# The first pair of heads in a fused attention and feed-forward kernel: an earlier projection, low parts read from the PSUM bank, two copies made by transfer, and the next pair's splits spread over four groups

## What is computed

```python
def _attn_ref(q, k, v, proj):                 # q, k, v: (2, 8, 768, 64), proj: (64, 6)
    q_bits = (np.einsum('bhsd,dk->bhsk', q, proj) > 0).astype(np.int64)
    k_bits = (np.einsum('bhsd,dk->bhsk', k, proj) > 0).astype(np.int64)
    powers = 2 ** np.arange(n_bits)
    q_bucket = np.sum(q_bits * powers, axis=-1)
    k_bucket = np.sum(k_bits * powers, axis=-1)
    mask = q_bucket[:, :, :, None] == k_bucket[:, :, None, :]
    scores = scale * np.matmul(q, k.transpose(0, 1, 3, 2))
    scores = np.where(mask, scores, -1000000000.0)
    attn = softmax(scores)                    # written out with max, exp and sum in the original
    return np.matmul(attn, v)

def reference(...):
    x = attention output as (B * S, H * D)    # (1536, 512)
    x = max(x @ w1, x @ w2, x @ w3) @ w_out
    h = x @ w_in
    return (h / (1 + exp(-1.702 * h))) @ w_out2
```

## Time and profile before

| | us |
|---|---|
| median of 3 runs | 678.75 |
| lowest, highest | 678.73, 679.58 |
| the profiled execution, its own time | 679.09 |
| its span, from the first to the last instruction | 677.3 |
| mean granted clock of TensorE | 0.997 |

### The profile page before, as it was taken

How to read it: one execution, slowest core, us unless ns; L and a number is a source line. 1 busy time by engine, 2 the same in 40 slices (tenths; PEclk the granted TensorE clock), 3 DMA queues, 4 the chain that set the end, 5 groups by cost and what they waited for, 6 DMA issues and landing times.

```text
span 677.3 us, 11910 instructions
## 1 busy us (share of the span) xinstructions
PE 664.4 (98%) x3867; PEld 575.4 (85%) x3867; DVE 494.7 (73%) x981; ACT 345.9 (51%) x758; POOL 473.0 (70%) x532
## 2 busy tenths in 40 slices
PE   7799999999999999999999999999999999999998
PEld 5677777777777789999999999998888989888886
DVE  5877778787878799869778952778777665555554
ACT  5777877777867731011102453456454555445433
POOL 4756746688876799977871628798888667777720
PEclk8999999999999999999999999999999999999999
DMA  5736638457253101111001200112222224221102
GB/s 139 168 85 158 147 87 184 120 128 166 64 140 119 32 4 44 48 32 31 24 27 45 94 0 32 63 62 66 89 80 80 63 66 152 63 63 62 40 23 94
DMA packets 58268, 53.97 MB, mean 80 GB/s; under 512 B 28608, under 2 KB 47200, under 8 KB 58208
## 3 DMA queue, kind: packets, MB, share of 16 engines
q1 hardware_dynamic: 56560, 52.82, 29.1%
q10 hardware_dynamic: 1648, 0.39, 0.3%
HBM read 32.51 MB, written 3.15 MB: 53 GB/s over the span
## 4 chain that ended last, share of the span: by engine, by line
PE 89%; POOL 5%; DVE 2%; DMA 1%; issue 1%; ACT 1%; ACTq 0%; DVEq 0%; POOLq 0%
PE psS L1434 10%; PE psO L1456 10%; PE psR L1442 9%; PE psR L1503 7%; PE psR L1504 7%; PE psR L1505 7%; PE psS L1503 6%; PE psS L1505 6%; PE psS L1504 6%; PE psS L1604 4%; PE psS L1603 4%; PE psS L1602 4%; POOL w_lo L690 2%; PE psR L1384 1%; POOL w_raw L681 1%
## 5 line engine op out<-in xcount | busy, mean ns | idle before, releaser
L549 POOL TENSOR_SCALAR probs<-probs,lone,inv 128x768 f32<-128x768 f32 x96 | 93.9, 985 | 62.2 <-DVE inv L1071 62.2
L690 POOL TENSOR_TENSOR w_lo<-w_raw,w_hi 128x256 fp32r<-128x256 f32 x96 | 79.7, 843 | 45.5 <-ACT w_hi L911 44.8
L1053 DVE TENSOR_REDUCE neg_max<-psS 128x1 f32<-128x768 f32 x96 | 91.1, 950 | 13.5 <-PE psS L1434 9.5
L757 ACT ACTIVATE probs<-psS,neg_max 128x768 f32<-128x768 f32 x96 | 86.5, 901 | 20.6 <-DVE neg_max L1053 20.6
L532 POOL TENSOR_SCALAR w_hi<-w_raw 128x256 fp32r<-128x256 f32 (+1 forms) x79 | 49.1, 625 | 49.7 <-PE psS L1505 28.4
L1442 PE MATMUL psR<-ident,probs 128*128 128x128 f32 x576 | 74.7, 273 | 3.1 <-POOL probs L549 1.1
L766 ACT ACTIVATE probs_t<-psR 128x384 f32<-128x384 f32 x128 | 59.6, 491 | 30.6 <-PE psR L1442 30.3
L1442 PEld LDWEIGHTS psR<-ident,probs 128*128 128x128 f32 x576 | 66.4, 140 | 7.8 <-POOL probs L549 4.4
L1456 PE MATMUL psO<-probs_t,v_raw 128*64 128x384 f32 x384 | 68.8, 494 | 0.0
L1299 DVE TENSOR_TENSOR v_raw<-psR,early 128x384 f32<-128x384 f32 x64 | 35.4, 552 | 31.9 <-PE psR L1505 31.6
L1304 DVE TENSOR_TENSOR v_raw<-v_raw,bits 128x384 f32<-128x384 f32 x64 | 50.3, 787 | 8.0 <-ACT bits L934 5.3
(11 more groups left out here) (268 smaller groups left out, 1878.6 us busy)
## 6 DMA issues: line engine op xcount, KB each, us to landing
w_raw<-in_moe_w_in SPq DMA_DIRECT2D x16, 512.0 KB, 3.3
w_raw<-in_moe_w_out SPq DMA_DIRECT2D x32, 256.0 KB, 2.7
w_raw<-in_moe_w SPq DMA_DIRECT2D x9, 512.0 KB, 3.8
h_lo<-w_hi SPq DMA_DIRECT2D x22, 192.0 KB, 3.3
h_hi<-w_hi SPq DMA_DIRECT2D x18, 192.0 KB, 3.5
w_raw<-in_q SPq DMA_DIRECT2D x16, 192.0 KB, 3.2
v_raw<-in_v SPq DMA_DIRECT2D x16, 192.0 KB, 2.5
stacks<-w_hi SPq DMA_DIRECT2D x16, 192.0 KB, 3.6
```

The costliest lines, as they stand in the source:

```text
L549: pool.tensor_scalar(probs[i % PROBS][:, :], probs[i % PROBS][:, :], lone[:, i % 6:i % 6 + 1], inv[:, i % 6:i % 6 + 1], ALU.add, ALU.mult) ...
L690: pool.tensor_tensor(in2_slot(w_lo, n, which), in2_raw(n, PARTS2[which]), f32(in2_slot(w_hi, n, which)), ALU.subtract).then_inc(in2_split, 1)
L757: act.activation(probs[i % PROBS][:, :].rearrange("p (a b) -> p a b", a=2), psS[i % 2][:, :, 0:HALF], ACT.Exp, bias=neg_max[:, i % 6:i % 6 ...
L1053: dve.tensor_reduce(neg_max[:, i % 6:i % 6 + 1], psS[i % 2][:, :, 0:HALF], AX.XY, ALU.min).then_inc(max_ready, 1)
```

## The change

- TensorE projects head 0 straight after turning it and after 12 warm matmuls (6 before, then behind head 1's turning). The warm-up at the start has 37 matmuls (30 before), the one ahead of scores 0 has 37 (15 before).
- VectorE makes the bits of head 0 ahead of its low parts, and reads the operand of both low parts of head 0 from the bank `psS[0]` and no longer from `qk_t`; the q part scales in the same instruction.
- ScalarE places the marks of head 0 before it copies head 1. Its two `first_hot` copies of head 1 are gone: two SyncE transfers copy the high halves from the LO stacks to the HOT stacks, and scores 3 waits for them (`first_placed`).
- The v loads of pair 0 and pair 1 are issued behind these two transfers.
- GpSimd splits heads 2 and 3 later: the high part of head 2 in group 1 (in group 0 before), its low part in group 2 (0), the high part of head 3 in group 3 (1), its low part in group 3 (1).
- In SyncE's list the marks of head 2 move ahead of head 3's high and low parts. They stand behind head 2's low parts and the load of head 5.

```diff
-    WARM_UP = 30
+    WARM_UP = 37
@@ sync
             for m in range(2):
                 load_qk(m)
-            load_v(0)
             load_qk(2)
             load_qk(3)
+            sync.wait_ge(dve_stacked, 4)
+            sync.dma_start(f32(stack(1, K_HOT)[0:D, :]), f32(stack(1, K_LO)[D:P, :])).then_inc(first_placed, 16)
+            sync.wait_ge(pool_stacked, 4)
+            sync.dma_start(f32(stack(1, Q_HOT)[0:D, :]), f32(stack(1, Q_LO)[0:D, :])).then_inc(first_placed, 16)
+            load_v(0)
             load_v(1)
             for p in range(1, PAIRS):
                 for m in (2 * p, 2 * p + 1):
                     if p + 1 < PAIRS:
                         load_qk(m + 2)
+                    if m == 3:
+                        place_marks(2)
                     place_hi(m)
                     place_lo(m)
                 for m in (2 * p, 2 * p + 1):
-                    place_marks(m)
+                    if m != 2:
+                        place_marks(m)
@@ gpsimd
-                    if st < 2 and p + 1 < PAIRS:
+                    if p > 0 and st < 2 and p + 1 < PAIRS:
                         make_qk_hi(2 * p + 2 + st)
                         make_qk_lo(2 * p + 2 + st)
+                    if n in (1, 3):
+                        make_qk_hi(2 + n // 2)
+                    if n in (2, 3):
+                        make_qk_lo(n)
@@ scalar
             first_hot(0, K_HOT, slice(D, P))
-            first_copy_qk(1)
             for j in range(2):
                 place_first(0, j)
-            first_hot(1, Q_HOT, slice(0, D))
+            first_copy_qk(1)
...
-                    first_hot(1, K_HOT, slice(D, P))
@@ vector
-                    dve.wait_ge(act_stacked, 8)
+                    dve.wait_ge(act_stacked, 6)
...
             first_k_hi(0)
-            first_k_lo(0)
             dve.wait_ge(marks_made, 10)
             make_first_bits(0)
+            dve.wait_ge(dve_stacked, 1)
+            dve.tensor_tensor(halves(stack(0, K_LO)[0:D, :]), psS[0][D:P, :, 0:HALF], halves(f32(stack(0, K_LO)[D:P, :])),
+                              ALU.subtract).then_inc(dve_stacked, 1)
             dve.wait_ge(pool_stacked, 1)
-            dve.tensor_tensor(stack(0, Q_LO)[D:P, :], qk_t[0][0:D, :], f32(stack(0, Q_LO)[0:D, :]),
-                              ALU.subtract).then_inc(dve_stacked, 1)
+            dve.scalar_tensor_tensor(halves(stack(0, Q_LO)[D:P, :]), psS[0][0:D, :, 0:HALF], NEG_SCALE,
+                                     halves(f32(stack(0, Q_LO)[0:D, :])), ALU.mult, ALU.subtract).then_inc(dve_stacked, 1)
@@ tensor
-                    pe.wait_ge(act_stacked, 4 * a + 4)
+                    pe.wait_ge(act_stacked, (4, 6)[a])
+                    if a == 1:
+                        pe.wait_ge(first_placed, 32)
...
             first_turn(0)
-            keep_running(WARM_UP // 5)
+            keep_running(WARM_UP // 3)
+            first_project(0)
             first_turn(1)
-            first_project(0)
-            keep_running(WARM_UP // 2)
+            keep_running(WARM_UP)
```

More of the change, by code:

```diff
@@ L242, in lsh_attention_ffn @@
         dve_first = sem("dve_first")
+        first_placed = sem("first_placed")
         qk_loaded = [sem(f"qk_loaded{i}") for i in range(2)]
@@ L1121, in first_k_hi, with halves @@
                 dve.tensor_copy(stack(a, K_LO)[D:P, :], qk_t[a][D:P, :]).then_inc(dve_stacked, 1)
-            def first_k_lo(a):
-                dve.wait_ge(dve_stacked, (1, 4)[a])
-                dve.tensor_tensor(stack(a, K_LO)[0:D, :], qk_t[a][D:P, :], f32(stack(a, K_LO)[D:P, :]),
-                                  ALU.subtract).then_inc(dve_stacked, 1)
+            def halves(x):
+                return x.rearrange("p (j s) -> p j s", j=2)
             first_copy_qk(0)
             first_k_hi(0)
-            first_k_lo(0)
             dve.wait_ge(marks_made, 10)
             make_first_bits(0)
+            dve.wait_ge(dve_stacked, 1)
+            dve.tensor_tensor(halves(stack(0, K_LO)[0:D, :]), psS[0][D:P, :, 0:HALF], halves(f32(stack(0, K_LO)[D:P, :])),
+                              ALU.subtract).then_inc(dve_stacked, 1)
             dve.wait_ge(pool_stacked, 1)
-            dve.tensor_tensor(stack(0, Q_LO)[D:P, :], qk_t[0][0:D, :], f32(stack(0, Q_LO)[0:D, :]),
-                              ALU.subtract).then_inc(dve_stacked, 1)
+            dve.scalar_tensor_tensor(halves(stack(0, Q_LO)[D:P, :]), psS[0][0:D, :, 0:HALF], NEG_SCALE,
+                                     halves(f32(stack(0, Q_LO)[0:D, :])), ALU.mult, ALU.subtract).then_inc(dve_stacked, 1)
             first_copy_qk(1)
@@ L1149, in _ @@
                 if n == 0:
-                    first_k_lo(1)
+                    dve.wait_ge(dve_stacked, 4)
+                    dve.tensor_tensor(stack(1, K_LO)[0:D, :], qk_t[1][D:P, :], f32(stack(1, K_LO)[D:P, :]),
+                                      ALU.subtract).then_inc(dve_stacked, 1)
                 if n < GROUPS:
```

## The result

The changed kernel is slower by 0.28%: the ratio of its times to those of the kernel before is 1.0028, with a 95% interval of 1.0017 to 1.0039. The medians of 15 runs each are 681.38 us and 679.58 us, 1.8 us apart. The profiled execution took 681.83 us with a span of 680.0 us, against 679.09 us and 677.3 us; 2.7 us more in the span.

A forecast was written before the change was run, and what follows sets the result against it. TensorE, busy for 98% of the span, was taken to bound the kernel. Gap 3.1 us, less head gain 2.5 us, plus clock loss 1.4 us gave +2.0 us on the 678.75 us median: 680.75 us, range 679.0 to 682.2 us.

The forecast's parts named there:

- What bounds the kernel: Whole kernel: TensorE is busy for 98% of the span, and any wait behind 33 us adds to the time in full.
- The head up to scores 0: Start of the kernel: low parts from the bank at 0.95 us each, scores 0 at 10.85 us instead of 12.18 us.
- The second rival: Head 0's low parts take 1.46 us each, G is 1.5 us, +3.0 us in all, 681.75 us; chance 0.14.
- From scores 0 to the first sums: Head: exp 1 at 15.1 us instead of 17.43 us, first sums at about 16.1 us instead of 18.66 us.
- G: Time by which TensorE runs without a gap earlier, thanks to the faster head: 2.35 to 2.55 us, taken as 2.5 us.
- From the sums to the last wait: Behind the first sums: G of 2.5 us carried to TensorE's last wait, which ends near 30 us; no loss counted.
- Edits at nothing: Two transfers, later v loads, GpSimd's groups 0 and 3 without and with splits: costed at nothing, no gain beyond G.
- The new gap: Second pair of scores 12 waits for head 2's marks, landing at 42.5 us: 3.1 us (2.8 to 3.5).
- Head 3: Scores 15: head 3's marks land by 49.4 us, wanted at 49.5 us; just in time, 0 us.
- The clock: Behind the wait at scores 12: half clock for 3.4 us costs 0.8 to 1.5 us, taken as 1.4 us.
- The first rival: Scores 12 wait but the clock stays at full: +0.6 us, 679.35 us; chance 0.22.
- The third rival: Head 2's marks come in time for scores 12, the whole head is gained: -2.5 us, 676.25 us; chance 0.12.

The follow-up runs named there:

- the kernel with early splits: Changed kernel with GpSimd's splits of heads 2 and 3 back in groups 0 and 1, changed SyncE list kept; 0.9959 against the kernel before, span 675.1 us.
- the kernel with the filled gap: Changed kernel plus 50 warm bf16 matmuls ahead of the first pair of scores 12; 1.0013 against the kernel before, span 678.7 us.
- few warm matmuls: The kernel with early splits, but 6 warm matmuls between the turnings and 15 ahead of scores 0; 0.9955 against the kernel before, span 675.3 us.
- the first two experiments: Changed kernel with head 2's marks ahead of its low part: 1.0012; changed kernel with head 5's load behind those marks: 1.0006; both against the kernel before.

## Why the prediction was right

The forecast was +2.0 us and slower; measured are a ratio of 1.0028, which is +1.9 us, and +2.7 us in the profiled spans. The queue, which decides the direction, was forecast entry by entry. That +1.9 comes so near to +2.0 is partly luck: it is an average over executions with one stretch at half clock and with more, and the forecast described one with a single stretch, behind the new gap. By its steps:

- **What bounds the kernel.** Right. The waits that appeared behind 31 us went into the span in full, and where one was taken away its time came back, less what the next one took. Against the kernel with early splits the spans even grew by 0.5 to 0.9 us more than the booked waits and the half clock: 2.9 us for waits of 2.1 us, 3.5 for 2.6 us, and 4.9 us in the changed kernel for 2.8 + 1.6 us.
- **The head up to scores 0.** Scores 0 were to start at 10.85 us (the terms written down, 8.65 + 2.27, make 10.92) and started at 10.29 us. The turning of head 0 was over earlier: it started at 4.95 us as expected but took 0.85 us, where I had read its 1.1 us, with a wait in it, as its price. That half microsecond belongs to the execution and not to the change: in the kernel with the filled gap, which has the same head, the turning took 1.42 us and scores 0 started at 10.83 us. The prices of the low parts from the bank, 0.96 and 0.95 us, are those that I took. The second rival (1.46 us each) falls.
- **From scores 0 to the first sums.** Order and releasers as told: exp 1 at 14.64 us (15.1 predicted), sums at 15.66 us (16.1 predicted), released by exp 1. G at the sums is 3.0 us, where I counted 2.55 us. One holder I had not seen: scores 3 waited not for exp 1 but for GpSimd's marks of head 1. These took 1.83 us beside VectorE's low part of head 1, which has two SBUF inputs. Before the change they took 1.10 us from 15.76 us on, and VectorE began its low part only at 17.33 us. The chain that ended last does not pass through scores 3, so no cost of this in the time is shown.
- **From the sums to the last wait.** Here a term was missing. G falls from 3.0 to 2.18 us (2.5 predicted), because the clock was at 0.50 for 3.4 us from about 18.1 us on. On the chain, the three transposes of tile 1 ahead of scores 4 took 0.90 us and scores 4 took 1.29 us. In the kernel with the filled gap the clock did not fall and they took 0.55 and 0.72 us. Its head started 0.54 us later and its last wait still ended earlier, at 29.83 us: G was 2.46 us at the sums and 2.58 us at the end, nothing lost. From scores 0 to the end of the last wait it is 19.9 us with the fall and 19.0 us without, so the half clock cost 0.9 us here. I had said that no half clock comes up to scores 1, which held, and had looked no further.
- **Edits at nothing.** The two transfers, the late v loads and the emptied groups of GpSimd: no wait of TensorE names them. Norm 2 and norm 5 came earlier and gained nothing, as early splits show. That few warm matmuls do as well was not foreseen: I had counted the clock at full as their merit.
- **The new gap.** On the clock of the kernel before, the second pair of scores 12 came at 40.44 + 2.18 = 42.6 us (42.5 predicted), a gap of 3.2 us (3.1 predicted). Issues: 35.5 us for the low part (35.6), 40.6 us for the fourth issue of marks (40.6). The landing took 1.97 us behind that issue, where I took 1.8 us. The Trainium skill (DMA: Bandwidth & Descriptors, "Anatomy of one DMA — SWDGE (gpsimd) path") has a fixed 2.0 us for the other issuing path, and this one transfer of 18 KB comes within 0.03 us of it.
- **Head 3.** I had put its marks 0.1 us ahead of TensorE and charged 0 us. In the changed kernel that is right, since the gap and the clock made TensorE later still. But I treated it as a footnote, and it is half of the matter: with the first gap gone, scores 15 waited 1.7 + 0.4 us. My expectations for the first two experiments repeated the mistake.
- **The clock.** 1.4 us predicted, 1.6 us measured between kernels with and without the fall. The first rival, that the gap is there and the clock holds, does not describe the profiled execution. With the gap filled by warm matmuls it is what happens: ratio 1.0013.
- **The third rival** (the marks come in time) falls by the 2.8 us wait.

The sum with the measured terms: 3.2 + 1.6 - 2.2 = +2.6 us, against 2.7 us in the spans. The ratio of many runs is smaller, 1.9 us. The mean clocks say why in part: 9 of the 15 runs have one stretch at half clock and not two. Which of the two places is spared in them is not on record, and that part stays open.

## What to carry to other kernels

Before moving the producer of a transfer later, write down every entry of the issuing queue behind it with its issue time, add the landing, and compare with each consumer in turn, not only with the first: here two deadlines stood one behind the other at almost the same distance, and mending one gained little but what the clock gave back. Slack that an engine seems to have can be owed to a queue: here eight issues stood between GpSimd's low part and the landing that TensorE waited for. And a gap in a bound engine costs more than its length if the clock falls behind it; count both, and settle them apart by filling the gap with idle work.

## What the runs showed of the hardware that I had not expected

- A VectorE subtraction with two SBUF inputs and a GpSimd instruction cost each other time, and mostly the one that started second: two copies of 12 x 384, started 0.12 us behind VectorE, took 2.38 us beside it and 1.10 us beside the same subtraction from a PSUM bank. In the kernel before, where GpSimd's copy had started first (at 7.04 us), VectorE's low part took 1.46 us and not 0.95 us.
- The granted clock fell to 0.50 for 3.4 us in group 1 of the changed kernel, where TensorE worked in pieces (idle from 14.6 to 16.1 us, then short bursts), and not in an execution with the same instructions up to there. An idle stretch of 1.24 us with work on both sides left it alone, and so did 1.5 us at scores 12 and 1.7 us at scores 15, each in one execution; 2.8 us at scores 12 was followed by a fall in both traces that have it.
- The issue of one small transfer of marks holds SyncE for 0.7 to 0.9 us, as long as that of one of 192 KB (0.6 us) or longer, so that four of 18 KB cost the queue 3.3 us.
